# Decay table and query powers read from the partitions that hold the powers, in 16 transfers on two queues

## The reference

```python
batch, n_heads, seq, head_dim = (2, 8, 768, 64)       # block = 64
Dmask = np.where(rel >= 0, lam[:, None, None] ** rel[None, :, :], 0.0)   # rel = i - j in a block
lam_pow = lam[:, None, None] ** (pos[None, :, None] + 1)
for b in range(nb):
    intra = einsum('bhic,bhjc->bhij', qb, kb) * Dmask ;  intra = einsum('bhij,bhjd->bhid', intra, vb)
    inter = einsum('bhid,bhde->bhie', qb * lam_pow, kv_state)
    out[:, :, sl] = intra + inter
    kv_state = lam_block * kv_state + einsum('bhsd,bhse->bhde', kb * rev_pow, vb)
```

## Time and profile before

| | us |
|---|---|
| median of 3 runs | 458.53 |
| profiled execution, its own time | 459.72 |
| its span, first to last instruction | 457.9 |
| PE busy in the span | 438.7 |
| DVE / ACT / POOL busy | 268.2 / 151.9 / 147.0 |

### The profile page before, as it was taken

One profiled execution on the slowest core, in us unless ns is written; L12 is line 12 of the kernel. 1 busy time (PEld: TensorE's weight loads), 2 busy tenths in 40 slices (PEclk: granted clock), 3 DMA queues, 4 the chain that ended last, 5 costly groups with the idle time before them and its releaser, 6 DMA issues.

```text
span 457.9 us, 7070 instructions
## 1 busy us (share of the span) xinstructions
PE 438.7 (96%) x2892; PEld 420.1 (92%) x2892; DVE 268.2 (59%) x419; ACT 151.9 (33%) x284; POOL 147.0 (32%) x99
## 2 busy tenths in 40 slices
PE   6799859999999999999999999999999999999997
PEld 5688749989999999999999999999999999889985
DVE  1657993566835974643533424966565557999220
ACT  1154343065322141111524217344125134525312
POOL 1432536235523222332376422332422450600000
PEclk9899979999999999999999999999999999999999
DMA  6977810050220220202022022022022020001112
GB/s 209 320 219 269 289 67 2 1 183 20 73 94 0 93 77 16 92 1 94 1 93 92 1 92 94 0 93 92 1 92 93 0 93 2 0 1 70 69 47 92
DMA packets 14032, 37.05 MB, mean 81 GB/s; under 512 B 1576, under 2 KB 3120, under 8 KB 14000
## 3 DMA queue, kind: packets, MB, share of 16 engines
q1 hardware_dynamic: 14000, 36.60, 23.8%
HBM read 33.44 MB, written 3.15 MB: 80 GB/s over the span
## 4 chain that ended last, share of the span: by engine, by line
PE 87%; DVE 7%; DMA 3%; ACT 1%; issue 1%; SPq 1%; DVEq 0%
PE ps L550 10%; PE ps L552 9%; PE ps L573 9%; PE ps L572 9%; PE ps L571 9%; PE ps L551 9%; PE ps L489 3%; PE ps L657 2%; PE ps L656 2%; PE ps L655 2%; PE ps L433 2%; PE ps L408 2%; PE ps L634 2%; PE ps L635 2%; PE ps L636 2%; PE ps L444 2%
## 5 line engine op out<-in xcount | busy, mean ns | idle before, releaser
L741 ACT ACTIVATE hh<-ps 128x384 fp32r<-128x384 f32 x64 | 31.5, 492 | 173.1 <-PE ps L552 173.1
L1017 DVE SCALAR_TENSOR_TENSOR hl<-ps,hh 128x384 fp32r<-128x384 f32 x64 | 35.3, 556 | 83.3 <-ACT hh L741 83.3
L550 PE MATMUL ps<-cen_h,w1h_a 128*128 128x384 f32 x128 | 44.1, 344 | 0.5 <-DVE hl L1017 0.5
L550 PE MATMUL ps<-cen_h,w1h_b 128*128 128x384 f32 x128 | 44.2, 345 | 0.0
L552 PE MATMUL ps<-cen_h,w1l_b 128*128 128x384 f32 x128 | 43.1, 337 | 0.0
L552 PE MATMUL ps<-cen_h,w1l_a 128*128 128x384 f32 x128 | 43.1, 337 | 0.0
L573 PE MATMUL ps<-hh,w2l_b 128*128 128x384 f32 x128 | 43.1, 337 | 0.0
L572 PE MATMUL ps<-hl,w2h_b 128*128 128x384 f32 x128 | 43.1, 337 | 0.0
L571 PE MATMUL ps<-hh,w2h_b 128*128 128x384 f32 x128 | 43.1, 337 | 0.0
L551 PE MATMUL ps<-cen_l,w1h_a 128*128 128x384 f32 x128 | 43.1, 337 | 0.0
L551 PE MATMUL ps<-cen_l,w1h_b 128*128 128x384 f32 x128 | 43.0, 336 | 0.0
(11 more groups left out here) (179 smaller groups left out, 1045.5 us busy)
## 6 DMA issues: line engine op xcount, KB each, us to landing
raw_a<-in_mlp SPq DMA_DIRECT2D x16, 512.0 KB, 4.8
raw_b<-in_mlp SPq DMA_DIRECT2D x16, 512.0 KB, 4.4
chunks<-in_qkv SPq DMA_DIRECT2D x12, 512.0 KB, 5.5
chunks<-in_qkv SPq DMA_DIRECT2D x22, 256.0 KB, 4.9
out<-out_sb SPq DMA_DIRECT2D x12, 256.0 KB, 2.0
raw_a<-in_val SPq DMA_DIRECT2D x2, 512.0 KB, 4.5
raw_b<-in_out SPq DMA_DIRECT2D x2, 512.0 KB, 4.6
seq_c<-const_seq SPq DMA_DIRECT2D x1, 768.0 KB, 5.8
```

Source lines behind the costliest of these rows:

```text
L550: mm(bank, wh_, xh, start=r == 0, stop=False)
L741: nc.scalar.activation(hh[:, slot, j], ps[j][:, 0:TB], ACT.Relu).then_inc(s_hh, 1)
L1017: stt(hl[:, slot, j], ps[j][:, 0:TB], 0.0, hh[:, slot, j].bitcast(F32), ALU.max, ALU.subtract).then_inc(s_hl, 1)
```

## The change

The scratch in DRAM and the semaphore `s_rv` are gone. SP issues four transfers and ACT four, one for each head, which read the shifted rows of `decay` directly from the one partition of `rv` that holds the head's powers. ACT then issues eight more, one for each head, for the query powers; their source is one row, read 64 times. The two semaphores now count eight transfers each. `rv` moves to the second buffer of `probs`, and DVE's `mask(1)`, the first to write there, waits for all query powers (which ACT issues after its heads); `mask(0)` writes the first buffer and waits for the decay table as before.

```diff
-    rv_dram = nc.dram_tensor("powers_dram", (H, 2 * P), F32, kind="Internal").ap()
...
-            rv = probs[0:H, 0, 0:2].rearrange("h a t -> h (a t)")
+            rv = probs[0:H, 1, 0:2].rearrange("h a t -> h (a t)")
...
+        def powers_rows(h, at, step, rows, cols):
+            powers = rv[h:h + 1]
+            return bass.AP(tensor=powers.tensor, offset=powers.offset + at, ap=[powers.ap[0], [step, rows], [1, cols]])
+
+        def decay_head(queue, h):
+            queue.dma_start(decay[:, h, :], powers_rows(h, 1, 1, P, P)).then_inc(s_tab, 16)
+
+        def query_powers(queue, h):
+            hp, par = divmod(h, 2)
+            queue.dma_start(qpow[par * Dh:(par + 1) * Dh, hp], powers_rows(h, 0, 0, Dh, P + 1)).then_inc(s_tabq, 16)
...
             load_chunk(0)
             sp.wait_ge(s_pow, 2 + 7)
-            sp.dma_start(rv_dram, rv).then_inc(s_rv, 16)
+            for h in range(0, H, 2):
+                decay_head(sp, h)
             load(1, 0, 2, s_tin)
-            sp.wait_ge(s_rv, 16)
-            sp.dma_start(decay[:, :, :],
-                         bass.AP(tensor=rv_dram.tensor, offset=1, ap=[[1, P], [2 * P, H], [1, P]])).then_inc(s_tab, 16)
-            for par in range(2):
-                sp.dma_start(qpow[par * Dh:(par + 1) * Dh],
-                             bass.AP(tensor=rv_dram.tensor, offset=par * 2 * P,
-                                     ap=[[0, Dh], [4 * P, HP], [1, P + 1]])).then_inc(s_tabq, 16)
             load(1, 2, 3, s_kin)
...
                 if n == 1:
-                    act.wait_ge(s_tabq, 32)
+                    act.wait_ge(s_tabq, 16 * H)
...
+            act.wait_ge(s_pow, 2 + 7)
+            for h in range(1, H, 2):
+                decay_head(act, h)
+            for h in range(H):
+                query_powers(act, h)
             for n in range(N):
...
                 if n == 0:
-                    dve.wait_ge(s_tab, 16)
+                    dve.wait_ge(s_tab, 16 * H)
+                if n == 1:
+                    dve.wait_ge(s_tabq, 16 * H)
...
-            pool.wait_ge(s_tab, 16)
+            pool.wait_ge(s_tab, 16 * H)
...
                 if n == 1:
-                    pool.wait_ge(s_tabq, 32)
+                    pool.wait_ge(s_tabq, 16 * H)
```

More of the change, by code:

```diff
@@ L171, in program @@
         s_lam, s_seq, s_hid, s_cw = (sem(n) for n in ("s_lam", "s_seq", "s_hid", "s_cw"))
-        s_pow, s_rv, s_tab, s_tabq, s_set = (sem(n) for n in ("s_pow", "s_rv", "s_tab", "s_tabq", "s_set"))
+        s_pow, s_tab, s_tabq, s_set = (sem(n) for n in ("s_pow", "s_tab", "s_tabq", "s_set"))
         s_tin = [sem(f"s_tin{c}") for c in range(RING)]
```

## The result

The changed kernel takes 479.28 us (median of four runs, 478.91 to 479.49) against 458.62 us before on the same chip: a ratio of 1.0446, interval 1.0428 to 1.0464. It is 20.7 us slower; I had predicted 478.2 us. The profiled execution of after took 479.31 us with a span of 477.5 us; before, these were 459.72 and 457.9 us, so that both differ by 19.6 us. The traces thus have 1.1 us less of a loss than the medians, since the profiled execution of before lies 1.1 us above its median. One execution in a slow state, 1111.88 us in e1_two_groups, raises that run's median from 469.96 to 470.2 us; its ratio leaves it out.

The account below looks back on a forecast made before the run. PE's dense work, beginning at the scores of chunk 2, was taken as the bound. A start 18.0 us later plus 1.7 us of clock made +19.7 us, 478.2 us for the median; range 461 to 488 us, to hold 0.8.

Parts of the forecast that it names:

- What bounds the kernel: PE is dense from the scores of chunk 2 at 18.70 us; a shift there reaches the end one for one.
- The sum of +19.7 us: Whole kernel: +18.0 us for the later dense start and +1.7 us for the clock, giving 478.2 us for the median.
- the 2.03 us: SP's queue: time of three issues that go, part of 4.9 us of queue time ahead of chunk 2.
- The source: Table reads out of eight partitions run at 25.8 GB/s: 30.6 us, 20.3 for decay and 10.2 for query powers.
- The door: Shared access to the eight partitions: all 788 thousand bytes pass through one share of 25.8 GB/s.
- The rival of the two doors: Table reads: two partition sets work side by side, 15.3 us, 463 to 465 us; chance 0.22, partial overlap included.
- The query powers: Second mask's wait: they follow the decay table through the same share, land at 35.4 us, PE goes on at 36.7 us.
- the twelve issues of ACT: ACT's queue: 4.7 to 8.0 us from 3.46 us on, until 8.2 to 11.5 us, priced at nothing.
- The load of chunk 2: SP's queue behind four heads: lands at 33.6 us, up to 2 us more, so the second mask is last or nearly.
- The clock: Start of PE's dense work after a gap: 3.4 us at half the clock give up 1.7 us.
- The source that costs nothing: Table reads cost no more than before; SP's shorter queue gains 1.7 us (1.15 to 3.3), 456.8 us; chance 0.15.
- The fourth rival: Each one-partition transfer runs on one DMA engine, 25.8 GB/s, same price as the forecast; chance within the forecast's 0.58.

Follow-up runs that it names:

- e1_two_groups: Changed kernel with SP issuing decay heads 0 to 3, ACT heads 4 to 7, and ACT alternating sets for the query powers: 470.2 us, ratio 1.0238.
- e5_decay_direct: Changed kernel with only the decay table read out of the eight partitions, the query powers out of DRAM: 479.25 us, ratio 1.0440.
- e6_queries_direct: Kernel of e2_sixteen_from_dram with only the query powers read out of the eight partitions, the decay table out of DRAM: 467.51 us, ratio 1.0191.
- e8_powers_apart: Changed kernel with the powers in a buffer of their own, so the second mask need not wait for the query powers: 475.18 us, ratio 1.0354.
- e10_hidden_table_later: Kernel before with the first load of chunk 2 issued ahead of the Fourier stage's table: 458.89 us, ratio 0.9993.
- e11_no_hole: As e10_hidden_table_later, with chunk 1's keys also issued ahead of SP's wait for the scratch: 459.12 us, ratio 0.9994.
- e3_dram_on_act: Kernel before with its three transfers and DRAM scratch all issued and waited for by ACT: 464.88 us, ratio 1.0131.
- e2_sixteen_from_dram: Changed kernel with the powers written to DRAM first and the same 16 transfers, on the same two queues, reading them there: 464.94 us, ratio 1.0123.
- e4_kept_warm: Changed kernel with 51 more constant products on PE after the first scores and 16 after the first values product: 476.92 us, ratio 1.0391.

## Why the prediction was right, and where it was not

**What bounds the kernel.** Right. The start of the dense work moved by 17.8 us and the span by 19.6 us; from 44 us on PE is busy as before. The sum of +19.7 us met the 19.6 us of the traces; the 1.1 us between 478.2 and 479.28 us are what was taken off for the median of before, while the profiled execution of after lies at its median. (The three issues of the 2.03 us are four; the sum is right.)

**The source.** Right in kind, that few partitions are read slowly whatever the number of DMA engines, and the number for the decay table came: 4.85 + 20.3 = 25.2 us was forecast, 25.3 us measured. The door was not as forecast, one for all eight partitions. There are two, of 23 to 24 GB/s each, and they are read one behind the other, so that the forecast share (25.8 GB/s) is near the rate of either; from 14 to 16 us, at 46 and 54 GB/s, they overlap, and this makes up for the lower rate. That part is luck. The rival of the two doors was real as a mechanism, and lost by the order of the heads: both queues issue heads 0 to 3 first, as the prediction had held against it. The run with the other order gives 470 us, 5 us above what I had put to it (463 to 465 us), since there too the second mask waits for late query powers.

**The query powers.** Here the number was right and the reason wrong. The step that lets the query powers pass through the same door behind the decay table, for 10.2 us, had them landed at 35.4 us, and they came at 35.07 us; but e5_decay_direct has the same time with the query powers from DRAM, and e6_queries_direct shows that the slow source alone adds 2.7 us to them. The term that failed is the twelve issues of ACT, which were priced at nothing. I had taken them for 4.7 to 8.0 us of the queue, until 8.2 to 11.5 us; they took until 29.0 us. A queue that has issued reads from a slow source does not issue on: the four issues before them took 11.23 us, and the first of the eight query transfers was issued at 14.75 us; the last of them landed at 35 us. The sign that I had named for this, ACT late with its first copy, did not show: the copy waited 1.57 us for PE, and it was the transfers that were late. With the wait in the second mask that price is on the path: 3.8 us of the shift of the start (36.50 us, against 32.73 us without the wait in e8_powers_apart), and 0.9% of the time with the clock in it. By the scores of chunk 3 it is 4.79 us (44.08 against 39.29 us): 3.77 us of start and 2.45 us of clock, less 1.43 us for which PE without the wait stands for POOL. What comes last was foreseen, `mask(1)` on the query powers; its cause was not.

**The load of chunk 2.** 33.6 us was forecast. In the changed kernel it was issued at 24.80 us and landed 8.4 us later, at 33.2 us; in e8_powers_apart, where PE waits for nothing else, it is there at 32.7 us. Right.

**The clock.** The term was 1.7 us, and the loss in the dense work 2.45 us: the round from chunk 2 to chunk 3 ran at 1.2 GHz until its last part, at a granted clock of 0.64 on average. The term was too small by 0.75 us, and 0.65 us came back at the end of the attention, which was not forecast; that the two cancel is luck too.

**The rivals.** The source that costs nothing, with a fall to 456.8 us, did not come, but no run shows what it would give. With the tables out of DRAM the same 16 transfers give 464.9 us, since the new wait is there; but that run keeps the way through DRAM. Its query powers were there at 20.0 us; read 3.6 us sooner, as from 3.49 us on, they would have been there at about 16.4 us, ahead of chunk 2 (an estimate from these two rows). What the runs do show is that the wait can cost by itself, 4.1 us there, and that I had put no price on it. The gain ascribed to SP's shorter queue rested on chunk 2 alone being last. In e10_hidden_table_later and e11_no_hole PE hardly waits for that load or not at all, and the time is the same, since PE's own work on the first chunks, begun at half the clock, ends at 18.3 and 18.7 us; and where SP merely does not wait, in e3_dram_on_act, the tables come later and the kernel is slower. The fourth rival, one DMA engine for a transfer, does not stand: from 8 to 12 us at most eight decay reads are in flight, which would be a DMA share of about 0.50 at most, and it is 0.68; e1_two_groups doubles the rate with transfers of the same number and size; and e2_sixteen_from_dram has transfers of the same shape and lands the decay table at 12.5 us.

**What stays open.** Why the traffic has a share of 0.65 to 0.69 in the slow stretches and not 1.00 is not settled. Neither is why ACT's and SP's queues stand while a slow source is read, nor what the kernel would take with a source in SBUF that is spread over many partitions.

## What to carry to other kernels

A read that fans one partition's row out to 128 partitions was bound here by the place it is read from: 23 to 24 GB/s for a set of four partitions. So count the bytes that leave each set and not the bytes in all; if such a read must be, let the queues read from different sets at the same time (24 against 47 GB/s). When a transfer is moved to another engine's queue, ask what its issue waits for, and where a buffer is borrowed, what the wait that protects it adds to the path: the two made 4.1 us here even with the tables out of DRAM. The stall at the start of the dense stretch had three things close behind one another in the kernel before (a table, a load, the clock): moving the load alone gained nothing that can be told, and only with the clock held as well was there 0.2%. And when two traces of a long kernel are compared, look for stretches behind the change where the clock differs: 0.65 us of the 20.25 us came back in one of them.

## What the runs showed of the hardware

- Four partitions (0 to 3) gave 24 GB/s to sixteen DMA engines from 8 to 12 us, the next four, by the order of issue, 23 GB/s from 16 to 20 us, and two such sets together 47 GB/s (e1_two_groups), where the best spread traffic is 413 GB/s.
- A slow source holds up the queue that issues: the four issues of 64 KB took 10.28 us on SP and 11.23 us on ACT, and the loads of chunk 1, out of DRAM, behind them on SP another 10.45 us for three; the issues of e5_decay_direct for reads out of DRAM took 4.99 and 3.90 us while decay reads went on, and 0.62 to 0.95 us each from 23.95 us on.
- Transfers of two queues are served much in the order in which they are issued: 8 KB from ACT, issued at 3.48 us, landed at 9.85 us behind SP's loads (e3_dram_on_act), against 3.55 us for the same 8 KB on SP's queue behind three loads.
- After PE had been idle from 7.2 us, the granted clock was 0.90 from 8 to 12 us and 0.50 from 12 us on (1.2 GHz). In e4_kept_warm PE did constant products from 31.22 us on, for 3.95 us, and the scores at 35.97 us found it at full speed (1.16 us).
- The same work of PE had a clock of 0.55, 0.75 and 0.50 in before, after and e4_kept_warm at the end of the attention, and what followed it moved by 0.5 to 0.8 us with it.
